# Transposes moved by a step and one-tile experts interleaved in an attention, dense and mixture-of-experts kernel

## What is computed

```python
# 1. attention: batch 4, heads 8, sequence 576, head size 64
scores = q @ k.T / 8
decay = cum[:, None] - cum[None, :]           # cum = cumsum(log(clip(f)))
attn = softmax(where(causal, -1e9, scores + decay))
x = (attn @ v)                                # 2304 tokens x 512
# 2. dense layer, 512 -> 2048 -> 512
h = x @ w_in
g = where(h >= 1, h, where(h <= -1, 0, (h + 1) ** 2 / 4))
x = g @ w_out
# 3. eight experts, each token goes to one, weighted by its softmax value
for e in range(8):
    out[idx == e] = gate[idx == e] * (relu(x[idx == e] @ w1[e]) @ w2[e])
```

## Time and profile before

| | us |
|---|---|
| median of 3 runs | 872.05 (871.83 to 873.91) |
| the profiled execution, its own time | 873.1 |
| its span, first to last instruction | 871.0 |
| PE busy | 843.6 (97%) |
| DVE, ACT, POOL busy | 418.2, 400.3, 361.5 |
| mean granted TensorE clock | 0.994 of full |

### The profile page before, as it was taken

The page is one execution under the profiler, slowest core; times in us unless marked ns, Lnnn a source line. Parts: engine busy times, 40 slices in busy tenths (PEclk is TensorE's granted clock), DMA queues, the critical chain, the costliest instruction groups (busy, mean ns, idle before and its releaser), DMA issues.

```text
span 871.0 us, 13892 instructions
## 1 busy us (share of the span) xinstructions
PE 843.6 (97%) x5082; PEld 789.4 (91%) x5083; DVE 418.2 (48%) x1002; ACT 400.3 (46%) x915; POOL 361.5 (42%) x366
## 2 busy tenths in 40 slices
PE   7999999999999999999999999999999999999995
PEld 4888888888999999999999999999998998998984
DVE  6677888887555544444445444455535110210201
ACT  6677777777566534434444444353332111211211
POOL 5755777884565411201201121074411492010384
PEclk9899999999999999999999999999999999999999
DMA  4767788884200121021021021342223354213140
GB/s 131 223 196 229 225 260 260 251 247 112 63 1 1 46 82 53 4 100 55 28 100 55 28 100 58 118 135 68 71 91 109 99 168 133 82 40 122 37 137 26
DMA packets 66335, 94.59 MB, mean 109 GB/s; under 512 B 6662, under 2 KB 42502, under 8 KB 66256
## 3 DMA queue, kind: packets, MB, share of 16 engines
q1 hardware_dynamic: 58160, 79.43, 30.4%
q10 hardware_dynamic: 6336, 9.44, 3.0%
q0 software_dynamic: 1760, 4.72, 1.4%
HBM read 69.82 MB, written 24.27 MB: 108 GB/s over the span
## 4 chain that ended last, share of the span: by engine, by line
PE 91%; ACT 3%; DVE 3%; issue 1%; DMA 1%; POOL 0%; SPq 0%; ACTq 0%; POOLq 0%
PE psum L1395 24%; PE psum L1397 24%; PE psum L1396 23%; PE psum L1369 6%; PE psum L1328 5%; PE psum L1353 5%; PE psum L1334 1%; DVE ptl L1045 1%; ACT pth L808 1%; ACT xo L814 1%; ACT pr L799 1%; PE psum L1338 1%; PE psum L1470 1%; PE psum L1454 0%; PE psum L1455 0%
## 5 line engine op out<-in xcount | busy, mean ns | idle before, releaser
L1395 PE MATMUL psum<-xh,winh 128*128 128x384 f32 x384 | 129.3, 337 | 0.7 <-ACT hpos L849 0.7
L1396 PE MATMUL psum<-xl,winh 128*128 128x384 f32 x384 | 128.4, 334 | 0.0
L1397 PE MATMUL psum<-xh,winl 128*128 128x384 f32 x384 | 128.4, 334 | 0.0
L1395 PE MATMUL psum<-gh,wouth 128*128 128x384 f32 x384 | 128.4, 334 | 0.0
L1397 PE MATMUL psum<-gh,woutl 128*128 128x384 f32 x384 | 128.3, 334 | 0.0
L1396 PE MATMUL psum<-gl,wouth 128*128 128x384 f32 x384 | 128.3, 334 | 0.0
L849 ACT ACTIVATE hpos<-psum,minus 128x384 f32<-128x384 f32 x96 | 55.9, 582 | 140.8 <-DVE hclip L1071 140.6
L1074 DVE TENSOR_TENSOR g<-hpos,hsq 128x384 f32<-128x384 f32 x96 | 66.8, 696 | 111.7 <-ACT hsq L851 111.7
L632 POOL TENSOR_TENSOR xst<-xst 128x384 f32<-128x384 f32 x24 | 24.3, 1012 | 176.5 <-DMA xst<-rinv_d 176.5
L799 ACT ACTIVATE pr<-pr,mmin 128x64 f32<-128x64 f32 (+2 forms) x144 | 81.6, 567 | 30.9 <-DVE mmin L1029 30.9
L1164 DVE SCALAR_TENSOR_TENSOR hl<-psum,hh 128x384 fp32r<-128x384 f32 x48 | 26.8, 558 | 139.5 <-ACT hh L882 139.5
(11 more groups left out here) (225 smaller groups left out, 1912.1 us busy)
## 6 DMA issues: line engine op xcount, KB each, us to landing
praw<-moe_w SPq DMA_DIRECT2D x48, 256.0 KB, 2.7
qraw<-q SPq DMA_DIRECT2D x16, 576.0 KB, 5.4
vraw<-vk SPq DMA_DIRECT2D x16, 320.0 KB, 3.0
xh<-yh_d SPq DMA_DIRECT2D x20, 256.0 KB, 4.1
xl<-yl_d SPq DMA_DIRECT2D x20, 256.0 KB, 4.4
kraw<-k SPq DMA_DIRECT2D x16, 288.0 KB, 4.3
c<-cum_d SPq DMA_DIRECT2D x32, 144.0 KB, 4.2
xa_d<-xo SPq DMA_DIRECT2D x16, 288.0 KB, 3.9
```

Source lines behind the costliest of these rows:

```text
L1395: nc.tensor.matmul(psum_at, ah, bh, start=start, stop=False)
L1396: nc.tensor.matmul(psum_at, ah, bl, start=False, stop=False)
L1397: return nc.tensor.matmul(psum_at, al, bh, start=False, stop=stop)
```

## The change

Four edits. **Fills**: fill 0 of a pair is done one step later (step 2), fills 2 to 5 one step earlier (steps 4 and 6), on PE, ACT and DVE alike. Fills 2 and 3 are put last in step 4, behind the late product. **Early product**: its two heads are done apart, head 0 at step 6 and head 1 at step 7; ACT's copy of the result goes from step 7 to step 8. **Singles**: the next single's first and second w1 halves, its transposes and the present single's products are interleaved: the transposes of single j + 1 now stand before the last three of the eight product groups of single j. **Buffers**: `h1h` and `h1l` have a second buffer each, in a part of `xh` and `xl` that is free by then.

```diff
+        over_x = [x[:, 1].rearrange("p k t -> p (k t)")[:, 0:KE * P].rearrange("p (f t) -> p f t", t=P)
+                  for x in (xh, xl)]
+        h1h, h1l = (h1h, over_x[0]), (h1l, over_x[1])
...
+        LATER = {0: 1, 2: -1, 3: -1, 4: -1, 5: -1}
+        BEHIND = (2, 3)
+        def fills_at(n):
+            at = [(n - FILL[k][0] - LATER.get(k, 0), k) for k in range(FILLS)]
+            return [(m // NB, k) for m, k in at if m % NB == 0 and 0 <= m < STEPS]
...
-                if i == 7 and 0 <= p < PAIRS:
+                if i == 8 and 0 <= p < PAIRS:
                     copy_early(p)
...
-            def relu_row(j):
+            def relu_row(j, h):
...
+            def high_one(j):
                 for h in range(2):
+                    act.wait_ge(h1_turned, 2 * j + h + 1)
+                    nc.scalar.copy(h1h[j % 2][:, 4 * h:4 * h + 4, :], psum[:, TURN1[h], :].rearrange(
+                        "p (f t) -> p f t", t=P)).then_inc(h1_h, 1)
...
                 with only_if(act, singles > j + 1):
-                    relu_row(j + 1)
...
+                    relu_row(j + 1, 0)
+                if j == 0:
+                    high_one(0)
+                with only_if(act, singles > j + 1):
+                    relu_row(j + 1, 1)
+                    high_one(j + 1)
...
                 p, i = tile_of(n)
-                if 0 <= n < STEPS:
-                    for k in fills_of(i):
-                        turn(p, k)
+                for p_, k in fills_at(n):
+                    if k not in BEHIND:
+                        turn(p_, k)
...
                 if i == 6 and 0 <= p < PAIRS:
-                    attend_early(p)
+                    attend_early_a(p)
+                if i == 7 and 0 <= p < PAIRS:
+                    attend_early_b(p)
                 if i == 2 and 0 <= p - 1 < PAIRS:
                     attend_late_a(p - 1)
                 if i == 4 and 0 <= p - 1 < PAIRS:
                     attend_late_b(p - 1)
+                for p_, k in fills_at(n):
+                    if k in BEHIND:
+                        turn(p_, k)
...
+            def single(j):
+                with only_if(pe, singles > j + 1):
+                    up_one(j + 1, 0)
+                if j == 0:
+                    pe.wait_ge(rows_ok, TT * (DENSE + 1))
+                    turn_one(0)
+                with only_if(pe, singles > j + 1):
+                    up_one(j + 1, 1)
+                if j >= 2:
+                    pe.wait_ge(rows1_ok, j - 1)
+                for f_ in range(KE - 3):
+                    down_one(j, f_)
+                with only_if(pe, singles > j + 1):
+                    turn_one(j + 1)
+                for f_ in range(KE - 3, KE):
+                    x = down_one(j, f_)
                 x.then_inc(down1, 1)
```

More of the change, by code:

```diff
@@ L553, in _ @@
                     sp.wait_ge(up1, 2 * singles)
+                    settle(sp, singles)
+                    sp.wait_ge(down1, singles)
                     settle(sp, singles)
@@ L828, in high_out @@
                 nc.scalar.copy(wouth[:, f_, :], woraw[:, f_, :]).then_inc(wo_h, 1)
-            for n in range(-AHEAD, STEPS + 1):
+            for n in range(-AHEAD, STEPS + 2):
                 if 0 <= n + 2 < STEPS:
                     exp(n + 2)
-                p, i = tile_of(n - 1)
-                if 0 <= n - 1 < STEPS:
-                    for k in fills_of(i):
-                        high(p, k)
+                for p, k in fills_at(n - 1):
+                    high(p, k)
                 p, i = tile_of(n)
-                if i == 7 and 0 <= p < PAIRS:
+                if i == 8 and 0 <= p < PAIRS:
                     copy_early(p)
@@ L1081, in _ @@
                     masked(n + 3)
[L1082 to L1086, removed]
+                for p, k in fills_at(n - 1):
+                    low(p, k)
+                    if k == FILLS - 1 and p >= 1:
                         copy_turned(p - 1)
@@ L1286, in single @@
                     part = slice(4 * h, 4 * h + 4)
-                    nc.vector.tensor_tensor(h1l[:, part, :], psum[:, TURN1[h], :].rearrange("p (f t) -> p f t", t=P),
-                                            h1h[:, part, :].bitcast(F32), ALU.subtract).then_inc(h1_l, 1)
+                    nc.vector.tensor_tensor(h1l[j % 2][:, part, :], psum[:, TURN1[h], :].rearrange("p (f t) -> p f t", t=P),
+                                            h1h[j % 2][:, part, :].bitcast(F32), ALU.subtract).then_inc(h1_l, 1)
             def expert(k, par, n, base):
@@ L1570, in full_group, with up_one, turn_one @@
                     out_rows(tt, par, at, first_piece, 1, hh, hl)
-            def up_one(j):
+            def up_one(j, h):
                 b = j % 2
-                pe.wait_ge(x1_in[b], 32 * (j // 2) + 32)
+                if h == 0:
+                    pe.wait_ge(x1_in[b], 32 * (j // 2) + 32)
                 at = slice(b * P, (b + 1) * P)
[L1576 to L1584, removed]
-                                  m == 0, m == KD - 1)
-                    x.then_inc(up1, 1)
-            def single(j):
-                b = j % 2
-                with only_if(pe, singles > j + 1):
-                    up_one(j + 1)
-                if j == 0:
-                    pe.wait_ge(rows_ok, TT * (DENSE + 1))
-                if j >= 2:
-                    pe.wait_ge(rows1_ok, j - 1)
+                if j < 2:
+                    pe.wait_ge(h3_l, KE * DENSE + h + 1)
+                else:
+                    pe.wait_ge(h1_ok, 2 * (j - 2) + h + 1)
+                pe.wait_ge(p_l, CR + PIECES * (j + 1) + KD * (h + 1))
+                for m in range(KD):
+                    x = three(psum[:, UP1[b][h], :], xh[:, 0, m, at], xl[:, 0, m, at],
+                              e_h[buffer_of(j)][:, KD * h + m, :], e_l[buffer_of(j)][:, KD * h + m, :],
+                              m == 0, m == KD - 1)
+                x.then_inc(up1, 1)
+            def turn_one(j):
                 for h in range(2):
```

38 lines of the change are left out of this document (19 added, 19 removed).

## The result

The changed kernel takes **879.25 us** (median of ten runs, 876.97 to 884.61) against 873.49 (871.83 to 876.56) for the kernel before: ratio **1.0072, 95% interval 1.0051 to 1.0093**. It is slower by 0.7%. The forecast was 870.8 with a range of 867.6 to 874.2, so it was wrong in its size and in its sign.

What follows compares the result with a forecast made beforehand. The prediction took PE, busy 97% of the span, as the bound, with only its waits to win. Attention -0.2, singles -3.0 and clock +2.0 gave -1.2 us, so 870.8 us, range 867.6 to 874.2.

Steps and rivals of the forecast that it cites:

- What bounds the kernel; the loss of 1.15 us a pair: PE is busy 97% of the span; waits at fills 6, 7 and 0 lose 1.15 us a pair.
- Fill 4 starts at T + 2.13 at best, a visible wait of 0.57: T ends step 4's late product; fills 2 and 3 start there, fill 4 loses 0.73 us, 0.57 of it visible.
- The denominators: VectorE's operation waits for Pool, ending at T + 5.41 with `combine_x`, T + 5.87 without; fill 0 loses 0.14 or 0.60 us.
- rival 2: Denominators miss the split of K and wait for Q's, 1.13 us in eight pairs: 877.9 us; chance 0.08.
- A pair then loses 0.73 + 0.16 + 0.14 + 0.05 = 1.08 us with combine_x: PE's waits at fill 4, fill 7, fill 0 and the late product, against 1.15 us a pair before.
- The rule that was weighed: VectorE in a two-port mode and GpSimd share a port pair; the later blocks. Otherwise the sum is 2 us lower.
- The clock, +2.0: PE's longer idle time ahead of 36.22 lets the clock fall to half afterwards, costing 2.0 us, bounds 1.5 and 3.0.
- The last pair (-0.4): Without scores, fill 4's new wait and the old ones cancel within 0.3; -0.4 us, including rounding in steady pairs.
- the one-tile experts (-3.0): In the singles, products cover the chain from transposes to `h1l`, removing 3.0 us of PE's waiting.
- rival 1: The clock does not fall after 36.2: -3.2 us, 868.9 us; chance 0.32.
- rival 3: The transposes' waits vanish, 12 us less, 857 to 859 us, needing the 2.13 us chain to shrink; chance 0.05.
- rival 4: ACT's and DVE's new order costs 0.3 us more in each of 12 pairs: +3.6, 874.4 us; chance 0.07.

Runs made afterwards that it cites:

- Experiment 11: Kernel of experiment 7 with the early product's first half ahead of fills 4 and 5, late product's copy ahead of low parts of fills 2 and 3: 860.48 us, ratio 0.9851.
- experiment 7: The changed kernel with only the denominators' operation moved ahead of the low parts of fills 4 and 5 on VectorE: 865.93 us, ratio 0.9915.
- experiment 9: The changed kernel with `kh` written twice behind each `combine_x`, 0.67 us of useless work on Pool: 869.47 us, ratio 0.9965.
- experiment 1: The kernel before with only the one-tile experts' part of the change: 869.66 us, ratio 0.9974.
- experiment 3: The kernel before with Pool's low part of Q ahead of its low part of K: 877.19 us, ratio 1.0059.
- experiment 10: Kernel of experiment 1 with the denominators' lines put ahead of the low parts' lines, which left VectorE's instruction order the same: 870.11 us, ratio 0.9968.
- experiment 2: The changed kernel with `xl` three steps later on VectorE (step 4 instead of 1): 877.55 us, ratio 1.0047.
- experiment 4: The changed kernel with Pool's low part of Q ahead of its low part of K: 881.82 us, ratio 1.0113.
- experiment 12: Kernel of experiment 7 with `xl` one step later on VectorE: 867.97 us, ratio 0.9957.
- experiment 5: The changed kernel with `combine_x` behind the splits of K and Q, `xh` and `xl` at step 4, load of x at step 5: 878.71 us, ratio 1.0063.
- experiment 6: Kernel of experiment 5 with the denominators ahead of the low parts of fills 4 and 5 on VectorE: 877.73 us, ratio 1.0042.
- experiment 8: Old order of fills with the one-tile experts' part, `combine_x` behind the splits, denominators planned ahead of low parts of fills 2 and 3: 881.24 us, ratio 1.0089.

## Why the prediction was wrong, step by step

- **What bounds the kernel; the loss of 1.15 us a pair: right.** Experiment 11 took most of it back with PE's own work unchanged.
- **Fill 4 starts at T + 2.13 at best, a visible wait of 0.57: right.** 0.56 in the pairs without `combine_x` and in experiment 7. In seven of the eight with it fill 4 waits 0.32 or 0.33, after 0.24 at fill 3, and starts at T + 2.35 (143.32).
- **The denominators: right without `combine_x`, half right with it.** They end with `kl` in the pairs without `combine_x` (91.81 + 0.82 = 92.63, `kl` 92.61), fill 0 waits 0.50, and a pair takes 13.0 against 13.1 forecast. In the others they start at T + 5.26 (146.23) and end at T + 5.42. The end is that of the forecast, T + 5.41, but they came 0.12 us later than worked out, half of the 0.24 that rival 2 needed, took 0.16, and so hardly waited. The meeting with `kl` is worth 13.0 - 12.54 = 0.46 a pair (experiment 9 has pairs of both kinds), the difference of 1.54 and 1.08 as reckoned. Taking the operation out of the path gave 0.2 more (12.34, experiment 7).
- **"A pair then loses 0.73 + 0.16 + 0.14 + 0.05 = 1.08 us with combine_x": the step that failed.** A pair of 12.6 was forecast, and 13.74 measured (14.17 in the first of the eight), 8.9 us more in eight pairs instead of 0.6 less. The sum stops at fill 0. `xl`, the third instruction behind the low parts of fills 6 and 7 on VectorE, was never costed: it stands in none of the rows and in no sentence. The forecast's own numbers led up to it: the cast of fill 6 at T + 6.16 and its low part 0.62 later, at T + 6.78, both as measured (147.14 and 147.74). In the trace of before the low parts of fills 6 and 7, `rturn` and the 320-column block take 1.41 us (105.79 to 107.20), which gives T + 8.19 for `xl`, and `ql` starts at T + 7.84. With no meeting the term holds: 12.53 to 12.60 a pair in experiment 9, against 12.6.
- **The rule that was weighed was the right one, in half its reach.** The forecast held it against the denominators' operation only. `xl` shows it for a VectorE instruction that reads two tensors of SBUF while Pool's operation is in progress: 2.76 us instead of 0.54 to 0.56 when it waits for nothing. The Trainium skill ("SBUF — State Buffer", Who interferes with whom) says this in a sentence of its own: "A DVE instruction with two SBUF inputs contends with a GpSimd instruction that reads SBUF". The trace agrees: the tensors of `xl` and those of `ql` are all in SBUF, and the 30 late starts above all stand until `ql` is done.
- **Rival 2: the right size by luck, the wrong mechanism.** It priced a missed meeting at 1.13 us in eight pairs, 877.9 in all, and the time is 879.25. But the denominators did not miss the split of K; `xl` met the split of Q. Its chance of 0.08 was for another meeting than the one that took place.
- **The clock, +2.0: half of its reasoning failed.** These rows of the changed kernel answer to the earlier trace rows:

```profile
20.40:27.20 6.80, 6.64 (x54) 6.04 (x54) 5.36 (x22) 5.72 (x19) 3.94 (x16) 1.00 0.71 216
...
35.20:42.00 6.80, 6.79 (x45) 6.54 (x45) 3.50 (x13) 3.98 (x13) 5.94 (x6) 0.75 0.73 223
```

  The clock did fall behind the idle time ahead of the third pair (3.36 us, to 35.21), as forecast (0.75 is a mean of full and half clock over the stretch). But the fall at 20.4 did not come, and the forecast counted the new one as if the old stayed. Over the whole start the change gained 0.5 us where +1.2 was reckoned. In the profiles of this study a fall before 36 us and one behind it mostly exclude each other, one profile a kernel, and no run shows why: experiments 1, 3, 10 and 11 have 0.50 to 0.55 in the early stretch and 1.00 behind, like the kernel before; the change and experiments 2, 4, 7, 9 and 12 have the reverse; 5, 6 and 8 have part of both. In experiment 7 the pair with the fall took 13.19, 0.86 more than the next.
- **The last pair (-0.4) and the one-tile experts (-3.0): right**, -0.4 and -2.9. The turns are followed by products without a gap:

```profile
854.66 1.03 PE L1618 MATMUL psum<-ident,hrow 128*128 128x128 f32 x8
```
- **Rivals 1, 3 and 4** did not happen. The order of ACT and VectorE (rival 4) costs nothing once `xl` is ahead of `ql`.

## What to carry to other kernels

When an edit moves work on an engine, follow that engine's list to the end of the period, not to the last instruction of interest, and write down for every instruction that shares a port with another engine how far ahead of its opponent it starts. A lead that is smaller than the shift you introduce (0.26 against 0.60 us here) is a term of the sum. Its size is what is left of the opponent's operation in progress at that moment: 0.2 us of `kl` before, 2.2 us of `ql` now. When a slower kernel shows one instruction several times longer, first move its opponent: 0.67 us of useless work on Pool gave back all of the 9 us, and moving the denominators one place gave 13.7 (1.57%). A move that changes when a buffer comes free has to be followed into the load queue too (experiment 2), and a load that is itself issued later has to be followed to its readers (5, 6 and 8). And before a run is called a test, see in its trace that the order did change (experiment 10).

## What was not expected of the hardware

- **Who is first decides, and the tie lies between 0.07 and 0.18 us.** `xl` was let through with a start 0.04 us behind the start of `ql` (experiment 7, 142.50 and 142.46, it took 0.54), once with 0.07 (experiment 12, 181.71 and 181.64, 0.54), and held with 0.18 (168.49 and 168.31 in experiment 12, it took 2.91). The records of Pool give starts this close only roughly.
- **The later one stands until the other is done, and the profile counts that as busy.** Held, `xl` grew by 2.2 us, and its end follows the end of `ql` wherever it starts. When `xl` went first, `ql` grew from 2.67 to between 2.98 and 3.16 (experiments 7 and 9), by most of the time of `xl`. The cheap order costs a fifth of the dear one, on an engine with idle time.
- **A periodic schedule can stay on such a tie.** In experiment 7 `xl` starts 0.02 to 0.05 us behind `ql` in four of the eight pairs and still goes through in all; in experiment 12 six pairs in a row take 13.2 to 13.5 and 12.0 in turn.
